# Expert layer and gated layer as one program part, with the expert's products alternating by weight group

## The reference

```python
# 1. attention with decay
state = f[:, :, t, :, None] * state + einsum('bhd,bhe->bhde', k_t, v_t)
y_t = einsum('bhd,bhde->bhe', q_t, state)
# 2. one of 8 experts for each token
logits = x @ w_gate + modality_bias[modality_id]
e_idx = argmax(logits);  gate_w = softmax(logits)[e_idx]
out[mask] = gate_w[mask] * (maximum(x[mask] @ w1[e], 0) @ w2[e])   # w1 384x1024, w2 1024x384
# 3. gated layer
xn = x / rms(x) * rms_g
out = (silu(xn @ w_gate) * (xn @ w_val)) @ w_out                   # 384x1536, 1536x384
```

## Time and profile before

| what | value |
|---|---|
| median of three runs | 909.58 us |
| the profiled execution's own time | 914.6 us |
| its span | 912.8 us |
| granted TensorE clock, mean | 0.977 |
| PE busy | 860.6 us (94%) |
| DVE / ACT / POOL busy | 53% / 42% / 17% |
| attention with routing | 0 to 194 us |
| expert tiles | 194 to 440 us |
| gated layer's first product | 447.6 us |

### The profile page before, as it was taken

One profiled execution on the slowest core, in us unless ns is written; L12 is line 12 of the kernel. 1 busy time (PEld: TensorE's weight loads), 2 busy tenths in 40 slices (PEclk: granted clock), 3 DMA queues, 4 the chain that ended last, 5 costly groups with the idle time before them and its releaser, 6 DMA issues.

```text
span 912.8 us, 15598 instructions
## 1 busy us (share of the span) xinstructions
PE 860.6 (94%) x5512; PEld 786.8 (86%) x5512; DVE 480.9 (53%) x753; ACT 384.3 (42%) x737; POOL 155.2 (17%) x154
## 2 busy tenths in 40 slices
PE   7999999489989989999799999999999999999996
PEld 7888888489889989999688888888888888888885
DVE  7899998477555466566244433333334333333331
ACT  4688886246444456465232331232232133122121
POOL 5324442511117600000000020010010002001001
PEclk9899999799999999999899999999999999999999
DMA  9668761495766877784200110010020000000000
GB/s 178 130 128 172 167 147 53 165 375 206 254 211 191 254 312 253 250 262 149 87 1 1 29 42 1 1 69 0 0 69 0 0 0 34 0 0 34 0 0 34
DMA packets 33263, 97.23 MB, mean 107 GB/s; under 512 B 7920, under 2 KB 24304, under 8 KB 29776
## 3 DMA queue, kind: packets, MB, share of 16 engines
q1 hardware_dynamic: 29392, 87.38, 32.3%
q0 software_dynamic: 3840, 9.47, 2.9%
HBM read 76.75 MB, written 20.08 MB: 106 GB/s over the span
## 4 chain that ended last, share of the span: by engine, by line
PE 50%; POOL 0%; ACT 0%; DVE 0%; issue 0%; ACTq 0%; DVEq 0%
PE g_ps L1551 6%; PE g_ps L1552 6%; PE acc_ps L1550 6%; PE g_ps L1550 5%; PE acc_ps L1552 5%; PE acc_ps L1551 5%; PE v_ps L1552 5%; PE v_ps L1550 5%; PE v_ps L1551 5%; PE xT_ps L1545 1%; POOL out L1448 0%; ACT x_hi L1463 0%; DVE x_lo L1503 0%; DVE h_lo L1529 0%; DVE hid L1519 0%
## 5 line engine op out<-in xcount | busy, mean ns | idle before, releaser
L1516 DVE TENSOR_TENSOR gs<-g_ps,sig 128x512 f32<-128x512 f32 x72 | 49.8, 691 | 180.9 <-ACT sig L1473 180.9
L1473 ACT ACTIVATE sig<-g_ps 128x512 f32<-128x512 f32 x72 | 43.1, 598 | 176.1 <-PE g_ps L1552 176.1
L1484 ACT CAST h_hi<-hid 128x512 fp32r<-128x512 f32 x72 | 44.6, 620 | 149.6 <-DVE hid L1519 149.6
L1550 PE MATMUL acc_ps<-wo_hi,h_hi 128*128 128x384 f32 x288 | 98.5, 342 | 0.2 <-DVE h_lo L1529 0.2
L1552 PE MATMUL acc_ps<-wo_lo,h_hi 128*128 128x384 f32 x288 | 97.1, 337 | 0.0
L1551 PE MATMUL acc_ps<-wo_hi,h_lo 128*128 128x384 f32 x288 | 96.7, 336 | 0.0
L1295 DVE TENSOR_TENSOR w_lo<-w_in,w_hi 128x768 fp32r<-128x768 f32 x52 | 59.2, 1158 | 67.2 <-ACT w_hi L1186 67.0
L1326 PE MATMUL h_ps<-x_hi,w_hi 128*128 128x256 f32 x312 | 89.0, 285 | 3.0 <-DVE x_lo L1279 3.0
L1327 PE MATMUL h_ps<-x_hi,w_lo 128*128 128x256 f32 x312 | 89.0, 285 | 0.0
L1328 PE MATMUL h_ps<-x_lo,w_hi 128*128 128x256 f32 x312 | 88.9, 285 | 0.0
L1551 PE MATMUL g_ps<-x_hi,wg_lo 128*128 128x512 f32 x216 | 85.9, 398 | 0.0
(11 more groups left out here) (192 smaller groups left out, 1797.7 us busy)
## 6 DMA issues: line engine op xcount, KB each, us to landing
w_raw<-in_w SPq DMA_DIRECT2D x13, 1536.0 KB, 7.3
w_in<-in_w SPq DMA_DIRECT2D x13, 1536.0 KB, 7.7
qkf_in<-in_qkf SPq DMA_DIRECT2D x46, 288.0 KB, 5.2
x_regions<-zero_row SPq DMA_DIRECT2D x14, 384.0 KB, 6.7
x_group<-x_regions SPq DMA_DIRECT2D x13, 384.0 KB, 3.4
y_sorted<-x_group SPq DMA_DIRECT2D x13, 384.0 KB, 6.1
v_in<-in_v SPq DMA_DIRECT2D x24, 192.0 KB, 4.3
g_in<-in_wg SPq DMA_DIRECT2D x3, 768.0 KB, 5.7
```

What stands on the lines that cost most here:

```text
L1473: nc.scalar.activation(sig[:], g_ps[:], ACT.Sigmoid).then_inc(sig_done, 1)
L1484: nc.scalar.copy(h_hi[:, fb % 2], hid[:]).then_inc(h_hi_done, 1)
L1516: nc.vector.tensor_tensor(gs[:], g_ps[:], sig[:], ALU.mult).then_inc(gs_done, 1)
L1550: nc.tensor.matmul(out, hi, rhs_hi, start=first, stop=False)
```

## The change: what it does

1. `mixture` and `gated_layer` become one function `experts` and one `Block`: no meeting of the engines between the layers. The three Blocks left are opened with `no_gpsimd_drain=True`.
2. w1 and w2 are loaded, rounded and subtracted in four groups each, of 384 KB (the list `PIECES` gives the order). Each group's raw buffer is loaded again as soon as that group is split, so raw weights arrive a tile ahead of their splitting.
3. PE alternates: hidden(0), hidden(1), then y of group 0, hidden(2), y of group 1, hidden(3), turn of the next x, y of groups 2 and 3. ACT and DVE split the weights of tile j+1 during tile j. h has two buffers in place of four in PSUM.
4. The y store of tile j-1 is issued right behind the x load, ahead of the weights.
5. The loop over tiles becomes a first tile, a loop over tiles 1 to 17 of which 1 to 11 are used, and a last tile, whose number is read from the table.
6. In the last tile the rows of block 0 are loaded (SP), squared (ACT, ahead of its h work), scaled, turned (two thirds behind hidden(3), one behind y of group 2) and split.
7. POOL starts the thirds only behind the first x split, each third in three instructions of 512 columns, and its 24 index writes (`by_token`) go four behind each third. Thirds 2 to 5 are rounded one tile later than before; w_out goes out in tile 7.
8. The warm-up products of PE ahead of the first tile go from 48 to 24.

```diff
+PIECES = ((1, 0), (1, 1), (2, 0), (1, 2), (2, 1), (1, 3), (2, 2), (2, 3))
-        block = ctx.enter_context(nc.Block())
+        block = ctx.enter_context(nc.Block(no_gpsimd_drain=True))
...
+        def tiles(eng, used, body):
+            body(0, "first")
+            with eng.Fori(1, MT - 1) as j:
+                with eng.If(j + 1 < used):
+                    body(j, "middle")
+            body(eng.value_load(table[0:1, LAST:LAST + 1], min_val=FULL - 1, max_val=MT - 1), "last")
...
+            def reload(j, e):
+                for which, g in PIECES:
+                    if which == 1:
+                        sp.wait_ge(w1_split, j * GR + g + 1)
+                        load_w1(e, g)
+                    else:
+                        sp.wait_ge(w2_split, j * GR + g + 1)
+                        load_w2(e, g)
...
+            load_w1(e0, 0)
+            sp.wait_ge(scattered, 16 * B)
+            load_x(0)
+            for which, g in PIECES[1:]:
+                (load_w1 if which == 1 else load_w2)(e0, g)
+            used = used_of(sp)
+            e1 = expert(1)
+            sp.wait_ge(x_landed, 16)
+            pad(e1)
+            reload(0, e1)
+            load_third(EARLY)
+            def body(j, place):
+                if place != "last":
+                    sp.wait_ge(x_turned, j + 1)
+                    load_x(j + 1)
+                if place == "middle":
+                    store_y(j - 1)
...
+                if place == "last":
+                    sp.dma_start(norm.token[:], by_token.rearrange("(n p) w -> p n w", p=P)).then_inc(token_in, 16)
+                    sp.dma_start(y_in[0], y_sorted[0:TB].rearrange("(q p) d -> p q d", p=P)).then_inc(y_landed[0], 16)
+                    store_y(j - 1)
+                    store_y(j)
...
+            pool.wait_ge(x_split, 1)
+            for i, (_, hi, lo) in enumerate(thirds):
+                pool.wait_ge(g_hi_done, i + 1)
+                for c in range(KD):
+                    last = nc.gpsimd.tensor_tensor(lo[:, cols], g_in[:, i % KD, cols], hi[:, cols].bitcast(F32), ALU.subtract)
...
+                if place == "last":
+                    act.wait_ge(norm_in, 16)
+                    square(0, 0)
+                hi_h(0)
...
+                pe.wait_ge(x_split, j + 1)
+                hidden(0)
+                hidden(1)
+                if place != "first":
+                    pe.wait_ge(y_kept, j * SUB)
+                gather_y(0)
+                hidden(2)
+                gather_y(1)
+                hidden(3)
+                if place == "last":
+                    turn(0, 0, 0)
+                    turn(0, 0, 1)
+                else:
+                    turn_x(j + 1)
+                gather_y(2)
+                if place == "last":
+                    turn(0, 0, 2)
+                gather_y(3)
```

More of the change, by code:

```diff
@@ new lines, in experts @@
+        xT_ps = ps("xTm_ps", [P, 4, TM])
+        pre_ps, cnt_ps = xT_ps[:, KD, 0:E], xT_ps[:, KD, E:2 * E]
+        xT2_ps = ps("xT2_ps", [P, 2, TB])
+        hv_ps = ps("h_ps", [P, 2, TB])
+        h_ps = hv_ps[:].rearrange("p s (i t) -> p s i t", i=2)
+        g_ps, v_ps = hv_ps[:, 0], hv_ps[:, 1]
+        y_ps = ps("ym_ps", [P, SUB, 512])
+        flat_ps = xT_ps[:].rearrange("p a t -> p (a t)")
+        acc_ps = [flat_ps[:, q * 512:q * 512 + DM] for q in range(2)] + [y_ps[:, q, 0:DM] for q in range(2)]
@@ L1109, in body @@
-                with only(sp, j, FIRST_BLOCK_AT + 1):
+                if place == "first":
+                    sp.wait_ge(rows_ready, 1)
+                if place == "middle":
+                    store_y(j - 1)
+                    with sp.If(j < WO_AT + 1):
+                        for i in range(KD, 2 * KD):
+                            with only(sp, j, i - KD + 1):
+                                load_third(i)
+                        with only(sp, j, WO_AT):
+                            sp.wait_ge(g_split, 2 * KD)
+                            sp.dma_start(g_in[:].rearrange("p k f -> p (k f)"), wo).then_inc(wo_landed, 16)
@@ L1200, in body @@
-                with act.If(j < 2 * KD - EARLY):
-                    for i in range(EARLY, 2 * KD):
-                        with only(act, j, i - EARLY):
-                            hi_third(i)
-            used_tiles(act, body)
+                    nc.scalar.copy(y_kept_rows[:, s], y_ps[:, s, 0:DM]).then_inc(y_kept, 1)
+                next_w2(3)
+                if place == "middle":
+                    with act.If(j < 2 * KD):
+                        for i in range(EARLY, 2 * KD):
+                            with only(act, j, i - 1):
+                                hi_third(i)
@@ L1207, in _ @@
+            blocks(act, body2)
         @block.vector
@@ L1308, in _, with three @@
+            blocks(dve, body2)
         @block.tensor
         def _(pe):
-            pe.wait_ge(marks, Routing.CHOSEN)
-            rt.count(nc, pre_ps, cnt_ps).then_inc(counted, 1)
-            pe.wait_ge(table_ready, 1)
-            for _ in range(WARM_UP):
-                nc.tensor.matmul(h_ps[:, 0, 0, 0:P], rt.ones_r[:], rt.ones_r[:], start=True, stop=True)
+            def three(out, hi, lo, rhs_hi, rhs_lo, first, last):
+                nc.tensor.matmul(out, hi, rhs_hi, start=first, stop=False)
+                nc.tensor.matmul(out, lo, rhs_hi, start=False, stop=False)
+                return nc.tensor.matmul(out, hi, rhs_lo, start=False, stop=last)
@@ L1555, in _ @@
-            for k in range(KD):
-                turn(0, 0, k)
+                    mm = nc.tensor.transpose(xT2_ps[:, k % 2, q * P:(q + 1) * P], y_in[par][:, q, k * P:(k + 1) * P], ident[:])
+                mm.then_inc(x2_turned, 1)
+            pe.wait_ge(marks, Routing.CHOSEN)
+            rt.count(nc, pre_ps, cnt_ps).then_inc(counted, 1)
+            pe.wait_ge(table_ready, 1)
+            used = used_of(pe)
+            for _ in range(WARM_UP // 2):
+                nc.tensor.matmul(hv_ps[:, 0, 0:P], rt.ones_r[:], rt.ones_r[:], start=True, stop=True)
```

679 lines of the change are left out of this document (337 added, 342 removed).

## The result

The changed kernel takes 898.05 us (median of 4 runs, 896.70 to 898.83), the kernel before 909.27 on the same chip: a ratio of 0.987, 95% interval 0.9854 to 0.9886. It is 11.2 us faster. The forecast was 889 (880 to 899), 20.3 faster: the direction and the range hold, but little more than half of the gain arrived. The profiled execution of the changed kernel took 896.7 us with a span of 894.8.

A forecast was written before the change was run, and what follows sets the result against it. PE was taken to bound the expert stage, its waits being winnable. Gated layer 22 us earlier plus 1.0 at Block ends: 914.6 - 23 = 891.6 profiled; between that and 886.6, 889 was forecast, range 880 to 899.

The forecast's parts named there:

- Ends of Blocks: Ends of three Blocks: leaving out POOL's drain gains 1.0 us (0 to 3).
- First expert product: Start of tile 0: less weight traffic ahead of x, first product at 189.2 (188 to 191), 4.7 us gained.
- Tile 0: First expert tile: a wait for tile 1's x rows, partly from POOL holding DVE; end at t = 22.5, 211.7.
- POOL never holds DVE: Tile 0 without POOL in the way: x wait of 1 to 2 us, tile end at t = 20.3.
- Tiles 1 to 11: Middle expert tiles: 17.63 us each plus 0.4 in all, ending at 406.0.
- the rival of a slower kernel: Expert tiles: x rows late in every tile, each delay feeding itself; about 935 us, chance 0.03.
- Last tile: Gap of 2.0 us (0.8 to 4.0) for skipped turns and table read, squares hold PE 1.1; stage ends 427.3.
- Behind 451.39 nothing changes but the end of the program: same instructions, same order.: Gated layer from its second product group on: unchanged except the program's end, only moved forward by 22 us.
- Profile against median: Whole kernel: the profiled run lay 5.0 us above the median; 889 taken between 891.6 and 886.6.
- clean tile 0: Tile 0: DVE never held, x of tile 1 in time, scatter early; 3 to 5 us less, 884, chance 0.14.
- full hold: Tile 0: POOL holds DVE for both thirds, end at t = 28; 5.5 us more, 895, chance 0.12.
- small waits: Third rival: small waits in every expert tile or late last-tile preparation; 6 to 11 us more, 898, chance 0.08.

The follow-up runs named there:

- e10: Kernel before, with 32 bytes of pad ahead of x2_hi and no GpSimd drain at Block ends: a gated step's 18 products 4.186 us, span 906.4.
- e8: Kernel before, with one pad of 32 bytes ahead of its weight buffers, shifting weights and x2 rows alike: a gated step's 18 products 4.123 us.
- e5: Changed kernel, with two pads of 96 bytes putting all large buffers back on multiples of 128: 898.77 us, a gated step's 18 products 4.177 us.
- e7: Changed kernel, padded so x2 rows, wo and h_hi lie on multiples of 128 bytes, gated weights 32 behind: a gated step's 18 products 4.200 us.
- e12: Changed kernel, unaltered, run again on one chip with e11 and the kernel before: 899.16 us, ratio 0.9866 to the kernel before.
- e11: e9 with the middle tile loop ending at the number of used tiles read from the table: 887.08 us, ratio 0.9733 to the kernel before.
- e6: Changed kernel, padded so g_in and gated weights lie on multiples of 128 bytes, x2 rows 64 behind: a gated step's 18 products 4.122 us.
- e9: Changed kernel, with 32 bytes of pad ahead of w1_raw, tile 1's rows loaded first and POOL's thirds later: 889.51 us, ratio 0.9762 to before.

## Why the prediction came out as it did

- **Ends of Blocks**, forecast 1.0 (0 to 3): 3.7 by e10. Under-sized and outside its bounds: 1.7 lie at the first two Blocks (1.1 by e8 against e5 to e7), 2.0 at the end of the program.
- **First expert product**, forecast 189.2 (188 to 191): 187.23. Of the 2.0 between them 1.6 are the first two drains (3.84 from attention's last copy to SP's first load, against 5.45), and 0.35 is attention, which ended sooner in this execution. x goes out at 180.50 (forecast 182.8, the same 2.0 in it). In the other traces without the drains the first product comes anywhere from 185.8 to 190.5.
- **Tile 0**, forecast end at t = 22.5, measured 25.1 (212.36 against 211.7). The wait for x rows behind the last w2 split is there, but its size has another source than the one that I weighed. The split ended at t = 9.9 and x went out at t = 11.5, as in my working without POOL (10.1 and 12):

```profile
195.35 1.81 DVE L1470 TENSOR_TENSOR w_lo<-w_in,w_hi 128x768 fp32r<-128x768 f32 x2
...
198.77 0.39 SPq L1119 DMA_DIRECT2D x_group<-x_regions  x1
```

  Then x needed 7.0 us to land (205.75, t = 18.5), where I had taken 3.4 to 4.4 for the data ahead of it and its own way. That is the term that I had too small. PE waited 5.53, the clock was down to 0.50 behind it, and the last two output groups took 5.37 in place of 4.2. In the other direction, the clock did not start low: the first two hidden groups took 4.41, where I had 6.05 (5.9 in most other traces of this start). The 22.5 lay between "POOL never holds DVE" (20.3) and "it holds it for both thirds" (28), and what came was neither: third 0 stretched two of DVE's parts by 1.1 us each and the split came in time all the same, and third 1 held DVE later, in a part of tile 1's weights. POOL so did both things that I had set against each other: in third 0 DVE gets in between the pieces (three pieces take 5.70 and DVE's parts 2.05), in third 1 it is held for all three:

```profile
187.45 5.70 POOL L1238 TENSOR_TENSOR wg_lo<-g_in,wg_hi 128x512 fp32r<-128x512 f32 x3 [10.07 <-DVE x_lo L1476]
...
199.50 3.72 POOL L1238 TENSOR_TENSOR wg_lo<-g_in,wg_hi 128x512 fp32r<-128x512 f32 x3
```

```profile
187.96 2.05 DVE L1470 TENSOR_TENSOR w_lo<-w_in,w_hi 128x768 fp32r<-128x768 f32 x1
191.91 2.05 DVE L1470 TENSOR_TENSOR w_lo<-w_in,w_hi 128x768 fp32r<-128x768 f32 x1
...
199.43 4.62 DVE L1470 TENSOR_TENSOR w_lo<-w_in,w_hi 128x768 fp32r<-128x768 f32 x1
```

  The Trainium skill ("SBUF — State Buffer", "Terms", shared port pair) has the pair locked for one instruction at a time. Third 0 agrees; the 4.62 in third 1, longer than the three pieces together, does not show a gap between them. In e12, the same kernel, third 1 takes 5.25 and DVE gets in (parts of 2.02 and 2.01), so this differs from one execution to the next.
- **Tiles 1 to 11**, forecast 17.63 each plus 0.4: 17.60 each (212.36 to 405.9), no wait. Right; the rival of a slower kernel found nothing to bite on.
- **Last tile**, forecast gap 2.0 (0.8 to 4.0): 2.95, within its bounds, with its cause now shown by e11. The squares held PE by 0.37 instead of 1.1. I had also read that an idle time of 2.35 or more costs 1.5 of clock; behind this one the clock stayed whole, and in e12 it cost 0.9. The stage ends at 427.7, forecast 427.3. That this came out to 0.4 is in part luck, since the parts cancel: start -2.0, tile 0 +2.6, tiles 1 to 11 -0.7, gap +0.8 (2.77 without the normal distance), last tile -0.3.
- **"Behind 451.39 nothing changes but the end of the program: same instructions, same order."** This is the step that failed. The instructions and their order are the same, the addresses are not, and each of the 1,296 products took 1.7% longer: 5.2 us, shown by e6, e9 and e11 (undone) and e10 (brought about in the kernel before). Nothing in my working priced a change of address.
- **Profile against median.** I placed the 5.0 us by which the profiled execution of before exceeds its median half in the change's favour. The miss of 9.1 by median splits so: 5.1 on the profile's own scale (896.7 against 891.6: pace +5.2, the first v_ps product +0.4, drain at the end -1.0, untraced +0.4), 2.6 from that placement (891.6 against 889), 1.4 because the changed kernel's median lies above its profile. What differs between executions of the kernel before I can show only in part, below.
- **The rivals.** A clean tile 0 (884), a full hold (895), small waits (898) and late rows (935) were all about the expert tiles, and none occurred: the time fell near the third by a cause that none of them named.

## What to carry to other kernels

"Same instructions, same order" is no proof of the same time: when a change shifts allocations by even 32 bytes, compare the distance between a product's two operands (here its remainder from 64) and the pace of one long row of products before and after, and try a pad if it differs. A loop bounded by the largest case costs each engine about half a microsecond for each skipped turn, at the very place where the next stage wants to start; end it at the number read from the table. When moving a load forward in a queue, ask what the load itself waits for, since everything behind it inherits that wait.

## What the runs showed of the hardware

The pace of fp32 products with 512 moving columns, at a granted clock of 1.00, is 229 ns each (4.121 / 18) or 233 (4.193 / 18) depending on where the operands lie; products with 384 columns take 2.12 / 12 = 177 ns. Only e10 moved the operands of these against each other, by the same 32 bytes, and they did not react (2.11).

In e8, a run of the kernel before but for its pad, one expert tile took 32.4 us (294.69 to 327.05), where tiles 1 to 11 take 17.6 to 21.7 otherwise. No semaphore holds PE there; it issues one product now and then, for over 10 us:

```profile
309.32 0.28 PE L1326 MATMUL h_ps<-x_hi,w_hi 128*128 128x256 f32 x1 [1.05 <-issue]
310.73 0.56 PE L1327 MATMUL h_ps<-x_hi,w_lo 128*128 128x256 f32 x1 [1.13 <-issue]
312.85 0.37 PE L1328 MATMUL h_ps<-x_lo,w_hi 128*128 128x256 f32 x1 [1.56 <-issue]
```

The busy time beside it, with the columns of the earlier trace rows:

```profile
300.00:305.00 5.00, 2.86 (x20) 2.62 (x20) 1.97 (x3) 0.60 (x1) 3.78 (x5) 1.00 0.57 228
305.00:310.00 5.00, 1.83 (x7) 0.91 (x6) 1.71 (x2) 1.31 (x2) 3.78 (x5) 0.97 0.35 38
310.00:315.00 5.00, 1.18 (x4) 0.93 (x4) 0.00 (x0) 0.00 (x0) 3.57 (x4) 0.50 0.76 308
```

PE, DVE and ACT starve, and the granted clock falls to 0.50, the lower of its two levels, after PE has been nearly idle. POOL does not: it goes on with its 24 index writes (`by_token`), one every 1.27 us, and PE issues its instructions in a row again from 317.09 on, 2.6 us behind the end of the last one:

```profile
313.51 0.97 POOL L1144 DMA_INDIRECT by_token<-of_token,pos  x1 [0.31 <-issue]
```

That instructions arrived late is not borne out: from 206 to 456 us the trace has no packet in the queues whose kind it calls `instruction`, only in these two:

```profile
q1 hardware_dynamic: 17052, 54.28, 63.0%
q0 software_dynamic: 768, 0.03, 0.2%
```

The index writes are a suspect, but not shown: the two other traces of this program have the same unbroken row of them and no such tile. The changed kernel makes the writes in fours, and in the eleven traces of it and its variants no tile from 2 to 10 took more than 18.0 us. Such a tile could be part of why the kernel before, and it alone, varies from chip to chip by up to 14 us; no trace shows that.
